# VectorE's side work in a seven-product MLP laid singly between its steps, with the second layer's weights split first and the first weight loads moved between the heads

## The reference, cut to what matters

```python
for t in range(S):                                  # 2 batches, 8 heads, S = 768, D = 64
    state = gamma * state + k[t] (x) v[t];  y[t] = scale * q[t] @ state
x = y as (B, S, 512)
xn = (x - mean(x)) / sqrt(var(x) + 1e-6) * g_ln
x = x + relu(xn @ w_ch1) @ w_ch2                    # w_ch1 512 x 2048, w_ch2 2048 x 512
logits = x @ w_gate;  w = softmax over the top 2 of 4 experts
for e in range(4):                                  # causal attention, Hd = 64
    a = softmax(causal(scale * (x @ wq[e]) @ (x @ wk[e]).T))
    out += w[:, e] * (a @ (x @ wv[e]) @ wo[e])
```

## Time and profile before

| | before |
|---|---|
| time, median of 3 (lowest to highest) | 492.82 us (492.19 to 495.42) |
| the profiled execution | 493.04 us, span 491.3 us |
| mean granted TensorE clock | 0.990 |
| PE / PEld busy | 455.9 / 405.7 us (93% / 83% of the span) |
| DVE / ACT / POOL busy | 321.7 / 219.6 / 293.2 us (65% / 45% / 60%) |
| chain that ended last | PE 56%, DVE 21%, POOL 10%, issue 5%, ACT 4%, DMA 2% |

### The profile page before, as it was taken

The page is one execution under the profiler, slowest core; times in us unless marked ns, Lnnn a source line. Parts: engine busy times, 40 slices in busy tenths (PEclk is TensorE's granted clock), DMA queues, the critical chain, the costliest instruction groups (busy, mean ns, idle before and its releaser), DMA issues.

```text
span 491.3 us, 8368 instructions
## 1 busy us (share of the span) xinstructions
PE 455.9 (93%) x2872; PEld 405.7 (83%) x2872; DVE 321.7 (65%) x669; ACT 219.6 (45%) x519; POOL 293.2 (60%) x391
## 2 busy tenths in 40 slices
PE   8998988989799798999789788999989999999997
PEld 7997877977698687888677677888889999999886
DVE  4654994386665763777586676454845878887964
ACT  2436644423424135523413423422434677777763
POOL 3654796676497289598376485763461255555740
PEclk9999998999999898999999999999999999999999
DMA  9989201211202202202211202410216234443314
GB/s 215 238 222 275 68 21 44 85 33 54 85 2 87 85 1 85 87 1 85 87 37 49 87 3 85 109 43 0 55 36 151 72 91 102 102 99 90 91 45 171
DMA packets 76521, 41.50 MB, mean 84 GB/s; under 512 B 48064, under 2 KB 70592, under 8 KB 76480
## 3 DMA queue, kind: packets, MB, share of 16 engines
q1 hardware_dynamic: 73824, 40.37, 30.8%
q10 hardware_dynamic: 2656, 0.60, 0.6%
HBM read 28.37 MB, written 3.15 MB: 64 GB/s over the span
## 4 chain that ended last, share of the span: by engine, by line
PE 56%; DVE 21%; POOL 10%; issue 5%; ACT 4%; DMA 2%; SPq 1%; POOLq 0%; DVEq 0%
PE ps L897 14%; PE ps L882 12%; PE ps L1002 7%; DVE rows L1564 6%; PE ps L1021 4%; PE ps L1036 3%; PE ps L1055 3%; ACT h_t_hi L1263 3%; DVE h_t_lo L1577 3%; DVE x L1572 3%; POOL w_lo L614 3%; PE ps L972 2%; PE ps L746 2%; PE ps L1079 2%; PE ps L736 2%
## 5 line engine op out<-in xcount | busy, mean ns | idle before, releaser
L1263 ACT ACTIVATE h_t_hi<-ps 128x384 fp32r<-128x384 f32 x64 | 31.3, 491 | 164.4 <-DVE ps L1596 67.5
L897 PE MATMUL ps<-w_hi,h_t_hi 128*128 128x512 f32 x192 | 77.0, 401 | 2.4 <-POOL w_lo L635 2.4
L897 PE MATMUL ps<-w_hi,h_t_lo 128*128 128x512 f32 x192 | 77.1, 402 | 0.0
L897 PE MATMUL ps<-w_lo,h_t_hi 128*128 128x512 f32 x192 | 76.8, 400 | 0.0
L1577 DVE SCALAR_TENSOR_TENSOR h_t_lo<-ps,h_t_hi 128x384 fp32r<-128x384 f32 x64 | 35.6, 556 | 60.6 <-ACT h_t_hi L1263 60.6
L699 POOL TENSOR_SCALAR a<-a,inv_den,weight 128x768 f32<-128x768 f32 (+5 forms) x48 | 33.9, 716 | 54.7 <-DVE inv_den L1813 28.8
L602 POOL TENSOR_TENSOR w_sum<-raw_w 128x256 f32<-128x256 f32 x30 | 23.9, 798 | 70.8 <-ACT raw_w L1196 70.8
L635 POOL TENSOR_TENSOR w_lo<-raw_w,w_hi 128x512 fp32r<-128x512 f32 x32 | 41.3, 1310 | 14.5 <-ACT w_hi L1211 14.5
L614 POOL TENSOR_TENSOR w_lo<-w_sum,w_hi 128x256 fp32r<-128x256 f32 x60 | 47.8, 807 | 2.5
L882 PE MATMUL ps<-xq_T_hi,w_hi 128*128 128x384 f32 x120 | 41.3, 344 | 6.0 <-DVE h_t_lo L1577 6.0
L882 PE MATMUL ps<-xq_B_hi,w_hi 128*128 128x384 f32 x90 | 31.7, 352 | 14.0 <-DVE h_t_lo L1577 14.0
(11 more groups left out here) (183 smaller groups left out, 1218.9 us busy)
## 6 DMA issues: line engine op xcount, KB each, us to landing
raw_w<-in_moe_w_ch SPq DMA_DIRECT2D x64, 256.0 KB, 3.2
k_twice_hi<-pj_hi SPq DMA_DIRECT2D x32, 96.0 KB, 2.2
k_twice_lo<-pj_lo SPq DMA_DIRECT2D x32, 96.0 KB, 2.2
out_y<-out_sb SPq DMA_DIRECT2D x12, 256.0 KB, 2.0
raw_k<-in_k SPq DMA_DIRECT2D x7, 384.0 KB, 5.3
raw_q<-in_q SPq DMA_DIRECT2D x7, 384.0 KB, 5.4
raw_v<-in_v SPq DMA_DIRECT2D x7, 384.0 KB, 4.5
q_both<-pj_hi SPq DMA_DIRECT2D x16, 96.0 KB, 2.1
```

The costliest lines, as they stand in the source:

```text
L897: mm = pe.matmul(acc_bank(tau), h_tile(a_, m, which)[:, u * P:(u + 1) * P], w2[b_][:, m % 2, part, :], start=(m % NG == 0 and which in ("1 ...
L1263: act.activation(h_tile("hi", m, part), part_bank(m, part), ACT.Relu).then_inc(s_hhi, 1)
```

## The change

- VectorE: `beside` gives way to `spare(m, slot)` with `SPARE`: six units a group, two ahead of `second_sum`, two behind it, one behind `h_t_lo` 11 and one behind `u3`; a unit is one transpose, one `add_heads`, two moments, `inverse` or `refine`. Token sums and low parts of half 1, the `centre` steps and `evict` are placed by four functions of their own. The order of differences and low parts in group 0 changes, and T1's and T4's low parts go into group 1.
- ScalarE: `w2_hi(m)` right behind `first_product(m)`; the splits of the first two groups one iteration earlier, w2's first last; order of `quad_hi` in groups 0, 7 and 8; `root(1)` one group later.
- GpSimd: `prepare_w2(m)` ahead of `prepare_w1(m + 1)`.
- SyncE: w1 of groups 0 and 1 behind `raw_q` of iterations 5 and 6, w2 of group 0 behind that of 7, w2 of group 1 behind all heads.
- Attention, on all three engines: `values(4)` ahead of `project_x2(0)`, `values(7)` ahead of `scores(0)`.

```diff
@@ -492,6 +492,21 @@
         @block.sync
         def _(sp):
+            def load_w1(m):
+                if m >= 2:
+                    sp.wait_ge(s_w1, weights_before(m - 1))
+                for half in range(2):
+                    cols = slice((m % NG + NG * half) * P, (m % NG + NG * half + 1) * P)
+                    sp.dma_start(raw_w1[:, m % 2, half], w1_rows[:, :, cols]).then_inc(s_w1raw[m % 2], 16)
+            def load_w2(m):
+                if m >= 2:
+                    sp.wait_ge(s_w2, 2 * (m - 1))
+                for half in range(2):
+                    sp.dma_start(raw_w2[:, m % 2, half], w2_rows[:, m % NG + NG * half, :]).then_inc(s_w2raw[m % 2], 16)
             def load_heads(it):
                 for n in "kqv":
@@ -501,19 +516,10 @@
                         else:
                             sp.wait_ge(s_scaled[n], 2 * (it - RB + 1))
                     sp.dma_start(raw[n][:, it % RB], heads[n][it]).then_inc(s_load[n][it % RB], 16)
-            def load_w(m):
-                f = m % NG
-                if m >= 2:
-                    sp.wait_ge(s_w1, weights_before(m - 1))
-                for half in range(2):
-                    cols = slice((f + NG * half) * P, (f + NG * half + 1) * P)
-                    sp.dma_start(raw_w1[:, m % 2, half], w1_rows[:, :, cols]).then_inc(s_w1raw[m % 2], 16)
-                if m >= 2:
-                    sp.wait_ge(s_w2, 2 * (m - 1))
-                for half in range(2):
-                    sp.dma_start(raw_w2[:, m % 2, half], w2_rows[:, f + NG * half, :]).then_inc(s_w2raw[m % 2], 16)
+                    if n == "q" and it in (HP + 1, HP + 2):
+                        load_w1(it - HP - 1)
+                    if n == "q" and it == HP + 3:
+                        load_w2(0)
             def load_qk(e):
@@ -547,11 +553,10 @@
                 if it == RB:
                     with nc.allow_non_contiguous_dma(reason="gain: 4 bytes a row"):
                         sp.dma_start(g_col[:, :], g_ln.rearrange("(k p) -> p k", p=P)).then_inc(s_gcol, 16)
-                if it == HP + 1:
-                    load_w(0)
-                    load_w(1)
+            load_w2(1)
             for m in range(2, GROUPS):
-                load_w(m)
+                load_w1(m)
+                load_w2(m)
             sp.wait_ge(s_xlo, len(X_ORDER))
             with nc.allow_non_contiguous_dma(reason="gate weights: 16 bytes a row"):
@@ -652,12 +657,12 @@
                 scale_pair(n)
             for name in FIRST_WEIGHTS:
                 weight_lo(0, name)
+            prepare_w1(1)
             prepare_w2(0)
-            prepare_w1(1)
             for m in range(1, GROUPS):
+                prepare_w2(m)
                 if m + 1 < GROUPS:
                     prepare_w1(m + 1)
-                prepare_w2(m)
             pool.wait_ge(s_wraw, 16 * (2 + E))
             pool.wait_ge(s_w2, 2 * GROUPS)
@@ -1127,15 +1132,15 @@
             values(3)
             turn_last(6)
             turn_last(7)
+            values(4)
             project_x2(0, range(KT))
             project_x2(1, range(KT))
-            values(4)
             values(5)
             project_x2(2, range(KT))
             values(6)
             project_x2(3, range(KT))
+            values(7)
             scores(0)
-            values(7)
             values(8)
             scores(1)
             values(9)
@@ -1236,15 +1241,15 @@
                     act.wait_ge(s_gcol, 16)
                 if it == HP + 1:
                     scale_w1(0)
-                if it == HP + 2:
                     for name in FIRST_WEIGHTS:
                         weight_hi(0, name)
+                if it == HP + 2:
+                    scale_w1(1)
+                    for name in ("A11", "A12", "A22"):
+                        weight_hi(1, name)
                 if it == HP + 3:
-                    scale_w1(1)
                     w2_hi(0, 0)
                     w2_hi(0, 1)
-                    for name in ("A11", "A12", "A22"):
-                        weight_hi(1, name)
             for it in (NIT - 2, NIT - 1):
                 y_out(it, 0)
             for it in (NIT - 2, NIT - 1):
@@ -1276,14 +1281,18 @@
             hidden_hi(0, "11")
             hidden_hi(0, "21")
+            hidden_hi(0, "22")
             quad_hi(0, "T2")
+            hidden_hi(0, "12")
             quad_hi(0, "T3")
-            hidden_hi(0, "22")
-            hidden_hi(0, "12")
             quad_hi(0, "T1")
             quad_hi(0, "T4")
             for m in range(1, GROUPS):
                 first_product(m)
+                w2_hi(m, 0)
+                w2_hi(m, 1)
+                if m == NG - 1:
+                    quad_hi(1, "B11")
                 if m == NG:
                     quad_hi(1, "B22")
                 if m + 1 < GROUPS:
@@ -1291,20 +1300,15 @@
                     weight_hi(m + 1, "A11")
                     weight_hi(m + 1, "A12")
                     weight_hi(m + 1, "A22")
-                if m == NG - 1:
-                    quad_hi(1, "B11")
                 hidden_hi(m, "11")
+                if m in (NG - 3, GROUPS - 1):
+                    root(m // NG)
                 if m == NG - 1:
                     quad_hi(1, "T2")
                     quad_hi(1, "B21")
-                if m in (NG - 3, GROUPS - 2):
-                    root(m // NG)
-                w2_hi(m, 0)
+                hidden_hi(m, "22")
                 if m == NG - 1:
                     quad_hi(1, "T3")
-                hidden_hi(m, "22")
-                w2_hi(m, 1)
-                if m == NG - 1:
                     quad_hi(1, "T1")
                 hidden_hi(m, "21")
                 if m == NG - 1:
...
@@ -1621,68 +1625,94 @@
                 dve.scalar_tensor_tensor(rows_tile(tau), acc_bank(tau).rearrange("p (k d) -> p k d", k=KT),
                                          rstd[:, tau:tau + 1], rows_tile(tau), ALU.mult, ALU.add).then_inc(s_x2, 1)
-            def beside(m, slot):
-                if m in (2, 3):
-                    for q_ in range(8 * (m - 2) + 2 * slot, 8 * (m - 2) + 2 * slot + 2):
-                        turn_rows(0, q_)
-                if m in (4, 13) and slot < 3:
-                    NORMS[m // NG][0](2 * slot)
-                if m in (5, 14) and slot == 0:
-                    NORMS[m // NG][1]()
-                if m in (5, 14) and slot == 3:
-                    NORMS[m // NG][2]()
-                if m == 5 and slot > 0:
-                    add_heads(1, slot)
+            SPARE = {0: (0, 1), 1: (2, 3), 2: (4,), 3: (5,)}
+            def spare(m, slot):
+                for unit in SPARE[slot]:
+                    if 0 <= 6 * (m - 1) + unit - 4 < NQ:
+                        turn_rows(0, 6 * (m - 1) + unit - 4)
+                    if 0 <= 6 * (m - NG - 1) + unit - 2 < NQ:
+                        turn_x2(0, 6 * (m - NG - 1) + unit - 2)
+                    if 0 <= 6 * (m - NG - 4) + unit < NQ:
+                        turn_rows(1, 6 * (m - NG - 4) + unit)
+                    if m == 4 and unit in (2, 3, 4):
+                        add_heads(1, unit - 1)
+                    if (m, unit) in ((4, 5), (5, 0), (5, 1)):
+                        NORMS[0][0](2 * ((unit + 1) % 6))
+                    if (m, unit) in ((14, 4), (14, 5), (15, 0)):
+                        NORMS[1][0](2 * ((unit + 2) % 6))
+                    if m in (5, 15) and unit == 2:
+                        NORMS[m // NG][1]()
+                    if m in (5, 15) and unit == 5:
+                        NORMS[m // NG][2]()
+            def before_second_sum(m):
                 if m == NG - 2:
-                    token_sum(1, T_ORDER[slot])
...
-                if m in (NG + 3, NG + 4):
-                    first = 8 * (m - NG - 3) + 2 * slot
-                    for q_ in range(first, first + 2):
-                        turn_rows(1, q_)
-            def group(m):
-                second_sum(m)
-                hidden_lo(m, "11")
-                beside(m, 0)
-                third_sum(m)
-                beside(m, 1)
-                fifth_product(m)
-                hidden_lo(m, "22")
-                beside(m, 2)
-                fourth_product(m)
-                hidden_lo(m, "21")
-                beside(m, 3)
-                last_product(m)
-                hidden_lo(m, "12")
-                if m == 5:
                     for b in range(B):
                         for kk in range(KT):
                             centre(1, b, kk)
+                if m == NG - 1:
+                    token_sum(1, "T4")
                 if m == NG:
+                    quad_lo(1, "T3")
+                    quad_lo(1, "T1")
+                if m == NG + 1:
                     for tau in range(U, NT):
                         evict(0, tau)
+            def behind_second_sum(m):
+                if m == 1:
+                    quad_lo(0, "T1")
+                    quad_lo(0, "T4")
+                if m == NG - 2:
+                    token_sum(1, "T1")
```

(49 more changed lines are left out.)

29 lines of the change are left out of this document (4 added, 25 removed).

## The result

The changed kernel takes **454.76 us** (median, 453.86 to 455.67) where the kernel before took 493.82 beside it: ratio 0.921 (95% interval 0.917 to 0.925). Its profiled execution took 455.67 us, with a span of 453.9. The page of the first: busy time of the engines, and the granted clock in 40 slices.

What follows compares the result with a forecast made beforehand. TensorE was taken to set the pace, losing time to VectorE results late at certain steps. Gains of 30.1 + 4.3 + 2.25 + 1.4 = 38.0 us off 493.04 gave 455.0 us, range 451 to 463.

Steps and rivals of the forecast that it cites:

- Groups, 30.1: Seven-product MLP, group 2's `u2` to group 15's: 205.4 us instead of 235.55, gain 30.1 us, bounds 24 and 31.
- The step on the norm: Group 5: with `refine` started at 9.05, `h_t_lo` 22 ends by 13.6 against 13.94 wanted, so nothing is lost.
- the 31.6 us of the prize: Groups 2 to 15: time lost between the measured 235.55 us and 13 gapless periods of 15.69, 203.97 us.
- w2's order, 2.4: MLP groups: splitting second-layer weights first removes TensorE's 2.4 us of waits for GpSimd's `w_lo`.
- Start, 4.3: Start of the seven-product MLP: group 2 starts at 87.95 instead of 92.29, gain 4.3 us, bounds 2 and 5.4.
- with differences and low parts at 0.94: MLP start, VectorE: at 0.94 us per operation, the last `h_t_lo` ends at 70.4 and group 1 starts about 71.3.
- Heads, 2.25: Head stage: fewer weight loads ahead of `raw_k` shorten the 9.40 us iteration; gain 2.25 us, bounds 0 and 2.5.
- Tail, 1.4: Attention: `values(4)` fills TensorE's wait before `project_x2(0)`; gain 1.4 us, bounds 0 and 1.5.
- the units fit: Denies this rival: in VectorE's windows single units don't quite fit, losing about 10 us, time 465; chance 0.12.
- start and heads did not stay: Denies this rival: MLP start gains only 2 and heads 0, time 459.5; chance 0.12.
- transposes ahead of `u2` are not on the path: Denies this rival: each of 48 transposes costs its 0.97 us in full, time 501.6; chance 0.01.
- the clock holds at 1.00: Denies this rival: TensorE's clock drops without pauses, groups take up to twice 15.69 us; chance 0.01.

Runs made afterwards that it cites:

- v_places: Changed kernel with single transposes elsewhere (groups 4 and 14 excepted): none ahead of `u2`, two behind it, one behind each of four later steps; 454.67 us.
- x_both: Changed kernel, GpSimd's first w2 split waiting for VectorE's two first-layer low parts, ScalarE doing group 1's first steps ahead of T3, T1, T4 splits; 453.89 us.
- u_w2: Changed kernel with the second layer's weights split last again, on ScalarE and GpSimd; 459.02 us.
- u_norms_w2: Changed kernel with half 0's root, heads and refinement back in group 5, centring behind it, and second-layer weights split last; 463.18 us.
- o_side: Kernel before with only VectorE's new placement in the groups and the second root one group later; 468.24 us.

## Why the prediction was right, and which terms were off

455.0 us was predicted (451 to 463), 454.76 measured. One thing in the working doesn't follow: the 450.5 to 458.5 "from the bounds of the terms". Those bounds add up to gains of 26 to 40.4 us, which is 452.6 to 467.0; the range on record was narrower than its terms. By stretch of the trace, the term on record, then found:

- **Groups, 30.1: 30.3** (235.55 to 205.23). No group over 15.69 but 5 and 6, which carry the mean's 1.3. The cost of the old placement held (20.2 against 20.7 by its undo); the reason for keeping them out from behind `h_t_lo` 22 and 21, a window of a third of a microsecond, did not (v_places). The step on the norm gave nothing to wait for, as said; but how the 31.6 us of the prize split was not understood: the 7.2 us of group 5 and the w2 waits were costed as separate things, and they share some 2 us (2.3 and 4.5 apart, 8.7 together). That the total came out owes something to luck: both were taken away, so how they share it did not matter.
- **w2's order, 2.4: 4.5 by its undo.** The row had only the waits that showed in the kernel before. One more, of 1 us, shows in group 1 once that group starts earlier.
- **Start, 4.3: 3.46** (29.42 us from the first hidden layer to group 2's first product, now 25.96). Group 1 took 16.71 where 15.6 + 1.05 was predicted, in two stops that cost 0.5 us each with the restart. What failed is the step "with differences and low parts at 0.94": from the start of the first hidden layer to group 1's first product it took 9.25 us instead of 8.43 (71.3 - 62.87), because two low parts ran at 1.90 and 2.04 beside the `w2_lo` that now stands there. For an operation beside GpSimd the prediction had 0.5 us, and took none at this place. With `w2_lo` cut in four it is 8.41 us, and x_both gets 0.62 us back by letting them run free.
- **Heads, 2.25: 2.45.** Undone it costs 3.6 (3.0 and 3.6 in the two executions at full clock), more than the stretch showed; the wait for `raw_q` and, in two executions, the clock are part of it, and how the rest splits is open.
- **Tail, 1.4: 2.1** by the traces, 1.5 by its undo (1.9 by the trace of that).
- The profiled execution started iteration 4 of the heads 1.20 us later than the one before (33.03 against the earlier trace rows's 31.83), the second profile of the same kernel 0.49 earlier: two executions of one kernel differ by 1.69 us there, so this is scatter, and with 0.30 gained in the last iteration the spans add up: -30.3 - 3.5 - 2.45 - 2.1 - 0.3 + 1.2 = -37.4.

The Trainium skill (SBUF — State Buffer, section SBUF: two separate sides) has VectorE, where it reads two tiles from SBUF, and GpSimd lock each other out for whole instructions. The traces agree: 0.17 us became 1.19 beside a step of 1.3, and shorter steps made the wait shorter. By that rule the prediction gave 0 to 3 us for the groups, by the row nothing; there it was nothing, with TensorE busy without a pause. Its price was 0.6 us at the start (x_both).

The rivals: the units fit (no group lost anything; v_places shows more room than was counted); start and heads did not stay; transposes ahead of `u2` are not on the path (VectorE idles 0.6 us behind them, and moving them changes nothing); the clock holds at 1.00 with TensorE busy without a pause from 87.28 us to the end of the groups.

What isn't measured by itself: the differences, low parts and evictions of groups 6 to 8. The undone parts sum to 20.7 + 8.7 + 3.6 + 2.6 + 1.5 = 37.1 of 38.6 us (493.13 to 454.52), so about 1.5 us are left for them, within the scatter of such a sum. Nor is there a run with a pair behind only one of the four steps.

## What to carry to other kernels

Where one engine paces and another is late at certain steps, look for how late each of its results may come, and lay the side work in pieces short enough for that: 48 transposes cost 20.7 us with a pair behind each of four steps in six groups, and nothing with one behind each of them and two behind `u2`, where VectorE would have waited anyway. Count the slack up to when the pacing engine wants the result, not up to when the late engine could go on. Price a stall with what may stand behind it too (the clock, here 1.5 us behind a stop of 2.7, but nothing behind one of 2.44), and look for the other engine's instruction beside a small operation that takes long: two causes that meet can cost more than their sum (here 8.7 against 6.8). An undo of one part therefore tells what it is worth now, not what it brought.

## What the runs showed of the hardware that I had not expected

- Operations of VectorE on 128x6 elements, 0.17 us free, took 0.86 and 1.19 us beside a GpSimd step of about 1.3 us that read and wrote SBUF; low parts of 128x768 took 1.90 and 2.04 instead of 0.95. With GpSimd's step cut in four they took 1.21.
- TensorE's granted clock fell behind stops of 2.70 us (0.66) and 3.10 us (0.64), and not behind one of 1.65 us in the same MLP (1.00). Length alone does not decide: it stayed at 1.00 behind 2.44 us in u_w2 and fell behind 2.45 us in o_side (0.66), 2.18 us in the kernel before (0.66 from 187.05 us on) and 1.69 us in the heads (0.72); and executions of one kernel differ (mean clock 0.995 to 1.000 in the four of u_w2). In u_norms_w2 it cost about 1.5 us: from group 5's `u2` to group 6's it is 22.98 us against 20.48, 1.05 of it the longer stop.
